# Attention steps moved to groups 0, 4, 7, 10 and 3, 6, 9, 12 of a tile, the next columns loaded behind the last store, and another order of the front's identity transposes

## The reference

```python
k_p = k.reshape(B, H, Sp, 8, D).mean(axis=3)          # Sp = 72
v_p = v.reshape(B, H, Sp, 8, D).mean(axis=3)
scores = scale * q @ k_p.T
attn = exp(scores - max(scores)); attn = attn / (sum(attn) + 1e-9)
x = attn @ v_p                                        # 4608 x 512
h = x @ w_in                                          # 512 x 2048
g = maximum(h, 0) + alpha * minimum(h, 0)
x = g @ w_out                                         # 2048 x 512
expert_idx = argmax(normed(x) @ normed(expert_emb).T / tau)
out[rows of e] = gate * (maximum(x[rows of e] @ w1[e], 0) @ w2[e])
```

## Time and profile before

| | us |
|---|---|
| median of 3 runs | 1513.42 (1511.84 to 1515.94) |
| the profiled execution, its own time | 1512.6 |
| its span in the profile | 1510.9 |
| PE busy | 1468.4 (97%) |
| POOL, DVE, ACT busy | 652.4, 782.6, 506.4 |
| mean granted TensorE clock | 0.99 of full speed |

### The profile page before, as it was taken

How to read it: one execution, slowest core, us unless ns; L and a number is a source line. 1 busy time by engine, 2 the same in 40 slices (tenths; PEclk the granted TensorE clock), 3 DMA queues, 4 the chain that set the end, 5 groups by cost and what they waited for, 6 DMA issues and landing times. The chain is left out here.

```text
span 1510.9 us, 21990 instructions
## 1 busy us (share of the span) xinstructions
PE 1468.4 (97%) x7769; PEld 1198.9 (79%) x7769; DVE 782.6 (52%) x1498; ACT 506.4 (34%) x873; POOL 652.4 (43%) x622
## 2 busy tenths in 40 slices
PE   7999999999999999999999999989999999999998
PEld 6787887887887877878878888868888888888886
DVE  5655667666666667666666576770002700055540
ACT  3333332222222232232232222534444444444442
POOL 4443234243243242342232242375455754566663
PEclk9999999999999999999999999999999999999999
DMA  7534122122131131120110122341111531025210
GB/s 206 171 112 164 28 61 87 37 69 85 37 90 50 44 105 40 53 79 29 50 50 15 36 91 70 139 154 44 43 47 38 201 101 47 31 93 194 94 70 11
DMA packets 67336, 119.53 MB, mean 79 GB/s; under 512 B 9756, under 2 KB 26140, under 8 KB 67104
## 3 DMA queue, kind: packets, MB, share of 16 engines
q1 hardware_dynamic: 59200, 99.20, 20.6%
q0 software_dynamic: 8032, 18.93, 3.9%
HBM read 92.34 MB, written 29.43 MB: 81 GB/s over the span
## 5 line engine op out<-in xcount | busy, mean ns | idle before, releaser
L1532 POOL TENSOR_TENSOR g_lo<-g_full,g_hi 128x512 fp32r<-128x512 f32 x144 | 187.5, 1302 | 560.3 <-ACT g_hi L1307 560.3
L717 PE MATMUL h_ps<-x_hi_in,weight_parts 128*128 128x512 f32 x1152 | 388.7, 400 | 2.2 <-DVE x_lo_in L989 2.2
L733 PE MATMUL y_ps<-weight_parts,g_hi 128*128 128x512 f32 x1152 | 359.9, 394 | 1.5 <-POOL g_lo L1532 1.4
L717 PEld LDWEIGHTS h_ps<-x_hi_in,weight_parts 128*128 128x128 f32 x1152 | 219.4, 190 | 49.5 <-issue 2.4
L733 PEld LDWEIGHTS y_ps<-weight_parts,g_hi 128*128 128x128 f32 x1152 | 212.8, 188 | 50.3 <-issue 4.8
L837 PE MATMUL y_ps<-weight_parts,x_hi_in 128*128 (+1 forms) x1032 | 244.5, 393 | 3.0 <-POOL x_hi_in L1583 3.0
L1307 ACT ACTIVATE g_hi<-g_full 128x512 fp32r<-128x512 f32 x144 | 90.9, 631 | 458.4 <-PE y_ps L733 398.8
L837 PEld LDWEIGHTS y_ps<-weight_parts,x_hi_in 128*128 128x128 f32 x1032 | 195.1, 190 | 44.7 <-issue 3.2
L717 PE MATMUL h_ps<-x_lo_in,weight_parts 128*128 128x512 f32 x576 | 227.2, 395 | 0.0
L733 PE MATMUL y_ps<-weight_parts,g_lo 128*128 128x512 f32 x576 | 224.3, 389 | 0.0
L1001 DVE TENSOR_SCALAR g_full<-h_ps,alpha 128x512 f32<-128x512 f32 x144 | 108.0, 750 | 220.3 <-PE h_ps L717 219.0
(11 more groups left out here) (188 smaller groups left out, 1714.2 us busy)
## 6 DMA issues: line engine op xcount, KB each, us to landing
shared<-in_w SPq DMA_DIRECT2D x8, 2048.0 KB
emb_all<-in_w SPq DMA_DIRECT2D x8, 2048.0 KB, 8.9
y_dram<-y_rows SPq DMA_DIRECT2D x9, 1024.0 KB, 5.0
shared<-in_q SPq DMA_DIRECT2D x34, 256.0 KB, 2.8
shared<-in_k SPq DMA_DIRECT2D x29, 288.0 KB, 2.8
shared<-in_v SPq DMA_DIRECT2D x29, 288.0 KB
x_dram<-shared SPq DMA_DIRECT2D x32, 256.0 KB, 2.3
y_rows<-x_dram SPq DMA_DIRECT2D x32, 256.0 KB, 4.6
```

What stands on the lines that cost most here:

```text
L717: mm = pe.matmul(h_ps[:, f % 2, :], w[:, k, f * P:(f + 1) * P], x[:, k, :], start=(n == 0), stop=(n == 3 * DC - 1))
L733: mm = pe.matmul(y_ps[:, j, :], a[:, f % 2, j * P:(j + 1) * P], w[:, f, :], start=(f == 0 and n == 0), stop=(f == FC - 1 and n == 2))
L1532: pool.tensor_tensor(gl[:, f % 2, :], g_full[:, f % 2, :], gh[:, f % 2, :].bitcast(F32), ALU.subtract).then_inc(gl_done, 1)
```

## The change

Three things are changed. The groups of the steps are now listed (`SCORES`, `VALUES`): tile 0 keeps its places, tiles 1 to 7 have the scores at 0, 4, 7, 10 and the values at 3, 6, 9, 12. SP issues `load_x(i + 1)` right behind the store of the last step (group 12, in tile 0 group 13) instead of at the end of group 13. In the front the 16 identity transposes ahead of the first step's transposes become 8 behind `scores(1)`; those of the later steps stand behind the step's own transposes, write `y_ps` and so wait for no copy; and ACT makes the first two weight chunks earlier.

```diff
-SPACE = 3
+SCORES = ((2, 5, 8, 11), (0, 4, 7, 10))
+VALUES = ((4, 7, 10, 13), (3, 6, 9, 12))
...
-        def step_at(i, f):
...
-            t, r = divmod(f - (2 if i == 0 else 0), SPACE)
-            return last_step(i) + 1 + t if i < NT - 1 and r == 0 and 0 <= t < FIRST else None
+        def step_at(i, f, slots):
...
+            at = slots[min(i, 1)]
+            return last_step(i) + 1 + at.index(f) if i < NT - 1 and f in at else None
...
         def sum_step(i, f):
-            return step_at(i, f - 1)
+            return step_at(i, f - 1, SCORES)
 
         def value_step(i, f):
-            return step_at(i, f - 2)
+            return step_at(i, f, VALUES)
...
                         store_x(s)
+                        if s == last_step(i + 1):
+                            load_x(i + 1)
...
-                    if f == 13 and i < NT - 1:
-                        load_x(i + 1)
...
-            keep_busy(WARM)
+            keep_busy(WARM, att[:, 0, 0:P])
             scores(0)
             scores(1)
-            for s in range(FIRST):
-                if s + 2 < FIRST:
-                    scores(s + 2)
-                if s:
-                    values(s - 1)
-                    pe.wait_ge(turned_copied, s)
-                keep_busy(WARM // 2 if s == 0 else WARM // 4)
-                pe.wait_ge(warmed, s + 2)
+            keep_busy(WARM // 4, att[:, 0, 0:P])
+            scores(2)
+            pe.wait_ge(warmed, 2)
+            turn_probs(0)
+            scores(3)
+            values(0)
+            for s in range(1, FIRST):
                 turn_probs(s)
-            values(FIRST - 1)
+                pe.wait_ge(shifted, 3)
+                keep_busy(WARM // 4, y_ps[:, 0, 0:P])
+                values(s)
+            pe.wait_ge(warmed, FIRST + 1)
...
                 exps(s)
+                if s == 2:
+                    w_hi(0)
                 if s >= 2:
                     x_out(s - 2)
                 if s:
                     copy_turned(s - 1)
-                if s >= 2:
-                    w_hi(s - 2)
+                if s == 2:
+                    w_hi(1)
```

More of the change, by code:

```diff
@@ L451, in last_step @@
             return TT * (i + 1) // QB - 1
-        def step_at(i, f):
-            t, r = divmod(f - (2 if i == 0 else 0), SPACE)
-            return last_step(i) + 1 + t if i < NT - 1 and r == 0 and 0 <= t < FIRST else None
+        def step_at(i, f, slots):
+            at = slots[min(i, 1)]
+            return last_step(i) + 1 + at.index(f) if i < NT - 1 and f in at else None
         def score_step(i, f):
-            return step_at(i, f)
+            return step_at(i, f, SCORES)
         def sum_step(i, f):
-            return step_at(i, f - 1)
+            return step_at(i, f - 1, SCORES)
         def value_step(i, f):
-            return step_at(i, f - 2)
+            return step_at(i, f, VALUES)
         def k_at(i, f):
@@ L874, in slot_layer2, with keep_busy @@
                 mm.then_inc(slots_done, 1)
-            def keep_busy(n):
+            def keep_busy(n, into):
                 for _ in range(n):
-                    mm = pe.transpose(att[:, 0, 0:P], c["ident"][:, :], c["ident"][:, :])
+                    mm = pe.transpose(into, c["ident"][:, :], c["ident"][:, :])
                 mm.then_inc(warmed, 1)
             pe.wait_ge(c["const_ready"], 2)
-            keep_busy(WARM)
+            keep_busy(WARM, att[:, 0, 0:P])
             scores(0)
             scores(1)
-            for s in range(FIRST):
-                if s + 2 < FIRST:
-                    scores(s + 2)
-                if s:
-                    values(s - 1)
-                    pe.wait_ge(turned_copied, s)
-                keep_busy(WARM // 2 if s == 0 else WARM // 4)
-                pe.wait_ge(warmed, s + 2)
+            keep_busy(WARM // 4, att[:, 0, 0:P])
[5 more added lines that the diff above has]
+            for s in range(1, FIRST):
                 turn_probs(s)
-            values(FIRST - 1)
+                pe.wait_ge(shifted, 3)
+                keep_busy(WARM // 4, y_ps[:, 0, 0:P])
+                values(s)
+            pe.wait_ge(warmed, FIRST + 1)
             pe.wait_ge(x_done, FIRST)
```

## The result

| us | before | changed |
|---|---|---|
| median | 1512.63 (1511.04 to 1515.94, 4 runs) | 1488.07 (1487.13 to 1490.19, 4 runs) |
| the profiled execution, its own time | 1512.6 | 1488.7 |
| its span | 1510.9 | 1487.0 |

The ratio is 0.9837, 95% interval 0.9816 to 0.9857. The change saves 24.5 us by the medians and 23.9 by the spans, where 26.4 were expected.

A forecast was written before the change was run, and what follows sets the result against it. PE, busy 97% of 1510.9 us, bounds the kernel; only its idle stretches and clock leave room. Terms 13.8 + 5.1 + 1.4 + 1.1 + 5.0 = 26.4 us off 1512.6, plus 0.8 for the median, give 1487.0 us; range 1483 to 1498.

The forecast's parts named there:

- The stall: First step of tiles 1 to 7: transposes moved to group 3 no longer wait for POOL's norm; gain 7 x 1.97 = 13.8 us.
- The clock: Behind three of the seven idle waits PE's clock falls; without the waits no falls, gain 3 x 1.7 = 5.1 us.
- clock falls anyway: Rival: small matmuls, not idle time, bring the clock down in the tiles; 21.3 us less, 1492; chance 0.15.
- The columns: Tile ends: next tile's columns load earlier, ACT never waits, PE's two waits for the low part go; gain 1.4 us.
- ring order: Rival: at tile ends the columns hold up value loads in tiles 1 to 5; 10 us at 2 a tile, 1497; chance 0.08.
- the full lateness would be paid: Value chunk queued behind the columns: by the skill's rule, at 2 us a tile, the sum would be 16.4, not 26.4.
- The router's choice: Tile 1: DVE ends 3.1 us sooner, so PE's 1.4 us wait shrinks to 0.3; gain 1.1 us.
- The front: Before the first large matmul: first values 2.5 us sooner, three steps save 2.5 together; gain 5.0 us, bounds 2.0 and 7.0.
- front hardly gains: Rival: ACT's chain or a transfer holds the front's steps; gain 2 instead of 5, 1490; chance 0.10.
- keep their distance: Later steps in tiles 1 to 7: transposes two groups after scores, a full group between, waiting for nothing; no cost.
- move along: Tile 0: keys and weight chunks are issued off the same events, so they come sooner with the front.

## Why the prediction was right

The forecast was 1487.0 us in a range of 1483 to 1498; the median is 1488.07, and all five terms have the right sign. The gain was 24.5 us instead of 26.4; the kernel before, measured again with one run more, was 0.8 faster than the 1513.42 from which the forecast started. The mechanism that carries most of the sum, the stall and the clock behind it, is shown by the runs. Two smaller terms came out less well than the total suggests. Term by term:

- **The stall, 13.8 us.** Right. The seven waits of 1.97 are gone, no first step waits at group 3, and PE comes to the transposes after the norm. The groups alone bring 22.2 us, which is more than this term and the clock's (18.9), since the next two terms belong to the groups as well.
- **The clock, 5.1.** Right in size. The profiles of two other kernels give 1.7 us a fall, and filling the same wait brought 5.7 (2.7 to 8.3). What the rows of one profile could not say is that a fall is a matter of chance (9 in 21); that this profile had three, the mean of these, was luck. The *clock falls anyway* rival is refuted by the fills: the small matmuls are all still there, and no fall comes in 7 filled or 63 unstalled places.
- **The columns, 1.4.** The waits are gone, but the step that credits the loads is wrong for this change. I read ACT's 4.72 us as the cause of PE's waits for `g_lo`, and it is one, since the earlier loads alone remove these waits. But the groups alone remove them as well, with ACT waiting for 3.1, and then tiles 1 to 7 take 707.85 us against 707.77 with everything. On top of the groups the columns are worth 0.1 us at most in these profiles. The *ring order* rival has a lateness (0.9 us) but not its price. The section of the Trainium skill that I cited for it ("DMA: Bandwidth & Descriptors", "Queues, rings and completion order") goes on to say that a later descriptor may finish its write before an earlier one. That a chunk "can't pass" and that "the full lateness would be paid" was my step and not the page's.
- **The router's choice, 1.1.** It was 1.4: the wait is gone. It varied from 0.4 to 2.4 in other kernels, so a tenth of a microsecond there was false precision.
- **The front, 5.0.** The 4.97 in the trace agrees by luck, twice. Inside the front, the first values came 3.3 us sooner where I had reckoned 2.5, and the three steps saved 1.6 where I had 2.5, since the clock fell in one of them. Between the kernels, this profile of before was at the lower clock from 12 to 19 us; with the same front the first large matmul started as early as 35.97 elsewhere. Over all profiles the gain is 3.8 us, of which 3.1 are left behind tile 0, and the front alone shows 2.9 by the medians. So the term was mis-sized, by one to two microseconds. By the medians the changed kernel is only 1.2 to 1.5 us ahead of the groups alone, on other chips, so the *front hardly gains* rival, with 2, is put further off by the marks but not excluded by the runs.
- **What the sum left out.** I held that the later steps "keep their distance" and "wait for nothing". For PE's own queue that was so; POOL's I did not go through for the last step, where `pool_values` of group 10 now stands ahead of the norm: 5 x 0.24 = 1.2 us. In tile 0 I wrote that keys and chunks "move along" with the front. In this profile PE waits 0.6 more for keys and 0.1 more for the norm, and over all profiles tile 0 is 0.8 us longer with the new front.

The 26.4 of the sum against 26.1 at the end of the tiles looks better than it is. Tiles 1 to 7 gained 21.6, and 13.8 + 1.4 + 1.4 − 1.2 = 15.4 of that are waits, which leaves 6.2 for three falls, where two other profiles show 1.7 a fall: 1.1 us have no cause that I could name. The front and tile 0 gained 4.5 in this pair of profiles and 3.1 over all of them. The fall near 940 us took 1.7 back. Without the luck in the front and the ill luck at the turn the sum is 21.6 + 3.1 = 24.7, an estimate from the marks, and the medians say 24.5.

## What to carry to other kernels

Where PE has to wait a microsecond or two, the price is the wait and, now and then, as much again in clock: read the granted clock behind each short idle stretch, over more than one profile. The same holds for a term that a pair of profiles seems to confirm: here the front's 5.0 was 3 to 4 over all of them. If the wait can't be moved behind other work, try filling it with transposes that depend on nothing and write to a free PSUM bank, and let the next large matmul find the clock up. It paid 2.5 us at the turn to the experts and about 4 in the front; more filling in the front alone gained nothing that the runs can tell. When a step moves to another group, list what stands ahead of it in the new group on every engine, since the one you don't list (here POOL) is where the new wait is.

## What the hardware showed that I had not expected

- The same idle 1.97 us between the same matmuls was followed by a fall of TensorE's clock from 2.4 to 1.2 GHz in 9 of 21 cases, and in different tiles from one execution to the next. Router waits of 2.1 and 2.4 us were each followed by a fall, one of 1.35 and one of 0.4 by none.
- Identity transposes whose result nobody reads held the clock as well as matmuls: without them the front ran at 0.50 from 12 to 43 us.
- A fall of about 3.4 us at half speed can come near 940 us in a stretch that nearly all the kernels here share: in 3 of 13 profiles, and in one of the two of the changed kernel. What decides it stays open.
